# Attention stage of a three-stage kernel: each k and v load takes one head of either pair and fills one run on all 128 partitions

## The chip, the cores and the metric

The kernel runs on one core of a Trainium2 chip. The metric is the device time of one execution in microseconds (us), from the launch of the program on the core to its end, taken as the median of several executions. All arithmetic is in float32; weights and activations of the large products are split into a high and a low part, each product being three matrix products.

## The reference, cut to what matters

```python
# q, k, v: (8, 8, 576, 64)   batch, head, sequence, head dim;   phi: (8, 8, 576, 32)
a = softmax(phi, axis=2)                       # over the sequence
k_m = einsum('bhsm,bhsd->bhmd', a, k)          # 32 memory rows per head
v_m = einsum('bhsm,bhsd->bhmd', a, v)
scores = (q @ k_m.transpose(0, 1, 3, 2)) / sqrt(64)
x = softmax(scores, axis=-1) @ v_m             # attention output, then (4608, 512)
h = x @ w_in;  x = (h * sigmoid(1.702 * h)) @ w_out        # 512 -> 2048 -> 512
# then: each of 4608 tokens goes to the best of 8 experts (512 -> 1024 -> 512),
# scaled by its gate probability and by a sigmoid output gate
```

## The kernel before, in words

Three stages follow each other. Stage A is attention, stage B the 512-2048-512 layer with the routing decision, stage C the experts. The change is in stage A alone.

Stage A works on 64 heads (8 batches of 8) in `NG` = 16 groups of `HG` = 4 heads. A group needs four inputs. `ph` is phi, 128 partitions of 576 floats. `qraw` is q, 128 partitions of 1152 floats. `kvm` holds k and v: its shape is `[128, 2, 2, 576]`, and its dimensions are partition, k or v (`w`), which head of a pair (`h2`), and 9 sequence rows of 64 floats (`CA * D` = 576). Partitions 0 to 63 hold heads 0 and 1 of the group (the first pair), partitions 64 to 127 hold heads 2 and 3 (the second pair). Of a head's 576 sequence rows, partition p of its half has rows 9p to 9p + 8, which lie side by side in memory: 2304 bytes. All three tiles exist twice (`u` = 0 or 1), so that group g + 2 is loaded into the buffers of group g once that group is through with them.

The loads are issued by SyncE, in program order, on one queue. For each group, `sp_group` (L456) first calls `load_phi` for group g + 2 (L415, it waits until DVE has transposed phi of the group that had the buffer, `s_phT`), then `load_qkv` (L420). `load_qkv` waits until the sums of group g are done (`s_kv`), issues two loads of k and two of v (L426), each with 64 partitions and two runs per partition, waits for the transposes of q (`s_qtr`), and issues the load of q (L429). Four chunks of w_in (L434) are loaded between the first groups. The semaphore of a `kvm` buffer rises by 16 per load, and by 64 per group.

On TensorE, `group` (L608) does this for each group: 18 transposes of the exponentials of phi (L619), the first four transposes of q (`q_part`, L605, which waits for q's load), then the 72 small products that sum k and v over the sequence (L631, which wait for the four loads of k and v), the output products of group g - 2 (L590), five more transposes of q, a transpose of the k sums (L639), and the scores (L649). ScalarE does the exponentials and the copies out of the accumulation memory and issues the stores of the attention output to `xT_scratch` (L887, one of 589,824 bytes per group). VectorE does the transposes of phi and of the scores, maxima, sums and normalisation. The engines are ordered by semaphores alone.

After group 15, SyncE's queue loads the first tile of x (L413) and the weight chunks of stage B, and stage B begins with the first product at L672. Stage B and stage C keep their own loads and are not touched.

Of the kernel before, what the change touches and what calls it, by code (L numbers as in the profile page):

```python
# [33 lines left out]
HG = 4  # L34
NG = B * H // HG
CA = 9
PA = S // CA
# [54 lines left out]
def build(nc, q, k, v, phi, w_in, w_out, w_gate, w_ogate, w1, w2, cst, out):  # L92
# [15 lines left out]
    with ExitStack() as ctx:  # L108
# [29 lines left out]
        with ExitStack() as a:  # L138
# [5 lines left out]
            qraw, kvm, ph = [], [], []  # L144
# [84 lines left out]
        s_kvl = [sem(f"kv_loaded{u}") for u in range(2)]  # L229
# [160 lines left out]
        def wait(eng, s, value):  # L390

            if not isinstance(value, int) or value > 0:
                eng.wait_ge(s, value)
# [15 lines left out]
        def _(sp):  # L409
# [10 lines left out]
            def load_qkv(g, b, u):  # L420

                wait(sp, s_kv, g - 1)
                for w, src in enumerate((k_v, v_v)):
                    for hh in range(2):
                        heads = src[bass.ds(g * HG + 2 * hh, 2)].rearrange("h (p c) d -> p h (c d)", c=CA)
                        sp.dma_start(kvm[u][hh * PA:(hh + 1) * PA, w], heads).then_inc(s_kvl[u], 16)  # L426

                wait(sp, s_qtr, 2 * (g - 1))
                sp.dma_start(qraw[u][:], q_v[bass.ds(g * P, P), :]).then_inc(s_q[u], 16)  # L429
# [11 lines left out]
            for dst, src in ((ident, "ident"), (mask, "mask")):  # L441
                sp.dma_start(dst[:], cst[src]).then_inc(s_cst, 16)
            load_qkv(0, 0, 0)
            load_phi(1, 0, 1)
            load_qkv(1, 0, 1)
            load_w(0, w_in_part(0, 0))

# [8 lines left out]
            def sp_group(g, b, r):  # L456

                u = r % 2
                if not isinstance(g, int) or g + 2 < NG:
                    load_phi(g + 2, b + 1, u)  # L460
                    load_qkv(g + 2, b + 1, u)

                if isinstance(g, int) and g + 1 < K1:
                    load_w(g + 1, w_in_part(g + 1, 0))
# [1179 lines left out]
```

## Time and profile before

| what | value |
|---|---|
| median of 3 runs | 1402.93 us |
| lowest and highest of them | 1402.65 and 1410.83 us |
| the profiled execution, its own time | 1402.57 us |
| span of its instructions | 1400.9 us |
| mean granted TensorE clock | 0.993 |
| first product of stage B (L672) starts at | 153.13 us |

The profile is of one execution on the one core. Its time is 1.67 us longer than its span, which is what lies before the first and behind the last instruction. Times in the rows are microseconds from the start of the span, unless they are marked ns. PE is TensorE, PEld its weight load, DVE VectorE, ACT ScalarE, POOL GpSimd, SPq, ACTq and POOLq the queues that issue DMAs. The DMA share is the mean busy share of the core's 16 DMA engines, and GB/s is what they moved; the records of an engine can overlap a little, so that a share can stand at 1.0 or just above.

### The profile page before, as it was taken

What the parts mean: (1) busy time and instruction counts of PE and PEld (TensorE: products, weight loads), DVE (VectorE), ACT (ScalarE), POOL (GpSimd) and SP (SyncE); (2) the same over time, 40 slices, a digit from 0 to 9 for tenths busy, and PEclk for the clock granted to TensorE, in tenths of its full rate; (3) what the DMA queues carried; (4) which work ended last, traced back from release to release, by engine and by line L of the source; (5) the groups of instructions that cost most, each with busy time, mean ns of one, the idle gap of its engine ahead of it and who ended that gap; (6) DMA issues with size and microseconds to landing.
All of it is one profiled execution on the core that took longest, in us unless ns stands there. A gap on an engine that the chain in (4) does not pass through costs nothing.

```text
span 1400.9 us, 26210 instructions
## 1 busy us (share of the span) xinstructions
PE 1351.8 (96%) x7922; PEld 1094.9 (78%) x7923; DVE 681.5 (49%) x1400; ACT 403.2 (29%) x725; POOL 517.7 (37%) x612
## 2 busy tenths in 40 slices
PE   5888899999999999999999999999999999999997
PEld 4566688888888888888888888887788888888885
DVE  4789633344353343433534344436655555555553
ACT  2455422222232232222322223223332222223221
POOL 1100486345443343433433334331434333433331
PEclk9999999999999999999999999999999999999999
DMA  9999635656556556465465654665784688649882
GB/s 229 290 325 313 234 100 168 194 200 194 181 191 183 179 169 182 171 187 175 160 183 176 179 192 147 184 189 203 236 257 119 164 254 249 185 115 261 246 237 61
DMA packets 164843, 275.31 MB, mean 197 GB/s; under 512 B 20179, under 2 KB 57316, under 8 KB 164788
## 3 DMA queue, kind: packets, MB, share of 16 engines
q1 hardware_dynamic: 104260, 197.16, 44.7%
q10 hardware_dynamic: 47408, 45.63, 12.7%
q0 software_dynamic: 13120, 31.82, 7.3%
q8 instruction: 31, 0.51, 0.2%
q14 instruction: 24, 0.20, 0.0%
HBM read 146.03 MB, written 100.45 MB: 176 GB/s over the span
## 4 chain that ended last, share of the span: by engine, by line
PE 86%; DVE 5%; DMA 3%; issue 3%; SPq 2%; ACT 0%; ACTq 0%; POOL 0%; DVEq 0%; POOLq 0%
PE ps L672 28%; PE ps L706 28%; PE ps L776 14%; PE ps L747 14%; DMA ph<-in_phi 1%; PE ps L716 1%; DMA qraw<-in_q 1%; SPq L426 1%; SPq L454 1%; PE ps L649 1%; DVE cmeta L1123 1%; DVE phT L1101 1%; DMA cq<-ch 1%; PE ps L631 0%; DMA cmeta<-record_scratch 0%
## 5 line engine op out<-in xcount | busy, mean ns | idle before, releaser
L672 PE MATMUL ps<-xs,W 128*128 (+1 forms) x1728 | 417.6, 391 | 1.1 <-DVE xs L1162 1.1
L706 PE MATMUL ps<-W,gs 128*128 128x512 f32 x1728 | 415.3, 390 | 0.1
L672 PEld LDWEIGHTS ps<-xs,W 128*128 128x128 f32 x1728 | 323.1, 188 | 72.0 <-issue 4.1
L706 PEld LDWEIGHTS ps<-W,gs 128*128 128x128 f32 x1728 | 324.3, 188 | 68.1 <-DVE gs L1217 0.8
L1215 DVE TENSOR_TENSOR gate<-ps,gate 128x512 f32<-128x512 f32 x144 | 99.6, 691 | 364.0 <-ACT gate L932 363.7
L932 ACT ACTIVATE gate<-ps 128x512 f32<-128x512 f32 x144 | 86.2, 598 | 471.3 <-PE ps L672 470.8
L776 PE MATMUL ps<-W,chT 128*128 (+1 forms) x936 | 218.3, 390 | 1.2 <-DVE chT L1348 1.2
L747 PE MATMUL ps<-W,cx 128*128 (+1 forms) x936 | 218.5, 390 | 0.5 <-issue 0.5
L1540 POOL CAST whi<-raw 128x512 fp32r<-128x512 f32 x128 | 81.3, 635 | 337.9 <-DMA raw<-in_moe_w 337.9
L776 PEld LDWEIGHTS ps<-W,chT 128*128 128x128 f32 x936 | 175.6, 188 | 38.3 <-issue 2.0
L747 PEld LDWEIGHTS ps<-W,cx 128*128 128x128 f32 x936 | 175.6, 188 | 37.3 <-issue 1.1
L1542 POOL TENSOR_TENSOR raw<-raw,whi 128x512 f32<-128x512 f32 x128 | 172.3, 1346 | 21.5 <-POOL whi L1540 20.0
L1217 DVE TENSOR_TENSOR gs<-gate,gs 128x512 fp32r<-128x512 f32 x144 | 120.4, 836 | 99.0 <-ACT gs L936 99.0
L340 POOL DMA_DIRECT2D crec<-record_scratch x160 | 90.0, 562 | 192.1 <-DMA out<-cy,cmeta 114.6
L936 ACT CAST gs<-gate 128x512 fp32r<-128x512 f32 x144 | 89.4, 621 | 115.1 <-DVE gate L1215 113.2
L997 ACT CAST chT<-cqT 128x512 fp32r<-128x512 f32 x41 | 25.2, 620 | 201.4 <-issue 159.8
L1348 DVE TENSOR_TENSOR chT<-cqT,chT 128x512 fp32r<-128x512 f32 x78 | 53.1, 691 | 38.9 <-ACT chT L997 37.6
L1312 DVE TENSOR_TENSOR cx<-cxT,cx 128x512 fp32r<-128x512 f32 x40 | 43.7, 1092 | 57.4 <-ACT cx L965 57.4
L1548 POOL DMA_INDIRECT record_scratch<-rec,posi x36 | 36.3, 1008 | 94.1 <-DVE posi L1277 85.7
L1597 POOL DMA_INDIRECT out<-cy,cmeta x39 | 43.1, 1106 | 70.5 <-ACT cy L1005 62.8
L1326 DVE TENSOR_SCALAR ch<-ps 128x512 f32<-128x512 f32 x37 | 25.5, 691 | 66.5 <-PE ps L747 66.3
L1335 DVE STREAM_TRANSPOSE cqT<-cq 128x512 f32<-128x512 f32 x78 | 50.6, 687 | 13.2 <-DMA cq<-ch 11.4
(158 smaller groups left out, 891.1 us busy)
## 6 DMA issues: line engine op xcount, KB each, us to landing
W<-expert_scratch SPq DMA_DIRECT2D x24, 2048.0 KB, 11.7
raw<-in_moe_w SPq DMA_DIRECT2D x128, 256.0 KB, 2.8
expert_scratch<-whi SPq DMA_DIRECT2D x128, 256.0 KB, 2.6
expert_scratch<-raw SPq DMA_DIRECT2D x128, 256.0 KB, 2.9
cq<-ch ACTq DMA_DIRECT2D x156, 128.0 KB, 3.9
crec<-record_scratch POOLq DMA_DIRECT2D x160, 64.0 KB, 5.6
kvm<-in_k SPq DMA_DIRECT2D x32, 288.0 KB, 5.2
kvm<-in_v SPq DMA_DIRECT2D x32, 288.0 KB, 7.0
```

Source lines behind the costliest of these rows:

```text
L340: eng.dma_start(crec[b * M:(b + 1) * M, r % 3], rows[:, b * P:(b + 1) * P].rearrange("(h n) d -> n h d", n=M)).then_inc(loaded, 16)
L672: mm = pe.matmul(ps[:, f % 2, :], W[:, col:col + P], xs[:, bass.ds(x0 + (x_lo * K1 + c) * T, T)], start=(c == 0 and w_lo + x_lo == 0), sto ...
L706: mm = pe.matmul(ps[:, 2 + s, :], gs[:, f % 2, g_lo, s * P:(s + 1) * P], W[:, col:col + DM], start=(f == 0 and g_lo + w_lo == 0), stop=(f ...
L747: mm = pe.matmul(ps[:, 3 * u + j, :], cx[:, u, x_lo, c, :], W[:, bass.ds(col, 512)], start=(c == 0 and x_lo + w_lo == 0), stop=(c == K1 - ...
L776: mm = pe.matmul(ps[:, 5 + r % 2, :], chT[:, r % 2, h_lo, c, :], W[:, bass.ds(col, DM)], start=(c == 0 and h_lo + w_lo == 0), stop=(c == C ...
L932: act.activation(gate[:, f % 2, :], ps[:, f % 2, :], ACT.Sigmoid, scale=QTOK).then_inc(b_sig, 1)
L936: act.copy(gs[:, f % 2, 0, :], gate[:, f % 2, :]).then_inc(b_ghi, 1)
L1215: dve.tensor_tensor(gate[:, f % 2, :], ps[:, f % 2, :], gate[:, f % 2, :], ALU.mult).then_inc(b_g, 1)
L1217: dve.tensor_tensor(gs[:, f % 2, 1, :], gate[:, f % 2, :], gs[:, f % 2, 0, :].bitcast(F32), ALU.subtract).then_inc(b_glo, 1)
L1348: dve.tensor_tensor(by_h(1, j), cqT[:, j * 512:(j + 1) * 512].rearrange("p (h c n) -> p h c n", h=2, n=M), by_h(0, j).bitcast(F32), ALU.su ...
L1540: pool.tensor_copy(whi[:, u, :], raw[:, u, :]).then_inc(e_hi, 1)
L1542: pool.tensor_tensor(raw[:, u, :], raw[:, u, :], whi[:, u, :].bitcast(F32), ALU.subtract).then_inc(e_lo, 1)
```

## The change

Each of the four loads of a group still moves 128 runs of 2304 bytes, 294,912 bytes in all. Before, a load was one pair: 64 partitions, and two runs (the pair's two heads) on each. Now a load is one head of either pair: the head `h2` of the first pair goes to partitions 0 to 63, the head `h2` of the second pair to partitions 64 to 127, one run on each partition. In `heads[h2]` the source's dimensions are, from the outside in, the pair (`a`, 2 of them), the partition of the pair's half (64) and the run (576 floats). The two pairs lie 73,728 floats apart, while 64 rows of 576 floats fill only 36,864, so that the outer two dimensions can't be read as one of 128. The data, the number of loads, the semaphores and the waits are the same.

```diff
                 wait(sp, s_kv, g - 1)
                 for w, src in enumerate((k_v, v_v)):
-                    for hh in range(2):
-                        heads = src[bass.ds(g * HG + 2 * hh, 2)].rearrange("h (p c) d -> p h (c d)", c=CA)
-                        sp.dma_start(kvm[u][hh * PA:(hh + 1) * PA, w], heads).then_inc(s_kvl[u], 16)
+                    heads = src[bass.ds(g * HG, HG)].rearrange("(a h) (p c) d -> h a p (c d)", a=2, c=CA)
+                    for h2 in range(2):
+
+                        sp.dma_start(kvm[u][:, w, h2], heads[h2]).then_inc(s_kvl[u], 16)
```

SyncE's queue in stage A, in the program before, the loads of group 0 and the first of group 1 (each row names the tile written, the input read, and partitions x runs x floats of the tile; x2 is two of them in a row):

```order
L418 DMA ph<-in_phi 128x576
L442 DMA ident<-const_ident 128x128
L442 DMA mask<-const_mask 128x128
L426 DMA kvm<-in_k 64x2x576 x2
L426 DMA kvm<-in_v 64x2x576 x2
L429 DMA qraw<-in_q 128x1152
L418 DMA ph<-in_phi 128x576
```

The same place in the changed program:

```order
L418 DMA ph<-in_phi 128x576
L443 DMA ident<-const_ident 128x128
L443 DMA mask<-const_mask 128x128
L427 DMA kvm<-in_k 128x1x576 x2
L427 DMA kvm<-in_v 128x1x576 x2
L430 DMA qraw<-in_q 128x1152
L418 DMA ph<-in_phi 128x576
```

No instruction has moved, on this engine or on another; only the form of the k and v loads differs, and the lines behind them are one higher.

## Rows read from the trace of the kernel before

**Rows 1.** The page: busy time by engine, and the chain that ended last.

```profile
PE 1351.8 (96%) x7922; PEld 1094.9 (78%) x7923; DVE 681.5 (49%) x1400; ACT 403.2 (29%) x725; POOL 517.7 (37%) x612
PE 86%; DVE 5%; DMA 3%; issue 3%; SPq 2%; ACT 0%; ACTq 0%; POOL 0%; DVEq 0%; POOLq 0%
```

**Rows 2.** Busy time of each engine in the two halves of stage A.

```profile
core 0: us, PE busy (x) PEld busy (x) DVE busy (x) ACT busy (x) POOL busy (x), PEclk, DMA share, GB/s
0.00:75.00 75.00, 50.81 (x950) 37.50 (x951) 46.32 (x102) 28.12 (x49) 11.34 (x18) 0.91 0.99 262
75.00:150.00 75.00, 65.05 (x1285) 45.35 (x1286) 66.74 (x151) 42.77 (x75) 0.00 (x0) 1.00 1.01 322
```

**Rows 3.** The chain that ended last, 30 to 75 us: start, length, what.

```profile
38.55 13.92 DMA qraw<-in_q
...
60.26 13.19 DMA ph<-in_phi
```

**Rows 4.** Timeline of SyncE's queue: start, length, line, transfer, count.

```profile
2.33 1.41 SPq L426 DMA_DIRECT2D kvm<-in_k  x2
...
99.48 1.43 SPq L426 DMA_DIRECT2D kvm<-in_k  x2
101.00 1.29 SPq L426 DMA_DIRECT2D kvm<-in_v  x2
102.54 0.38 SPq L429 DMA_DIRECT2D qraw<-in_q  x1
103.13 0.33 SPq L418 DMA_DIRECT2D ph<-in_phi  x1
107.44 1.43 SPq L426 DMA_DIRECT2D kvm<-in_k  x2
```

**Rows 5.** DMA issues in 0 to 150 us: count, size of each, median from issue to landing.

```profile
kvm<-in_k SPq DMA_DIRECT2D x32, 288.0 KB, 5.2
kvm<-in_v SPq DMA_DIRECT2D x32, 288.0 KB, 7.0
qraw<-in_q SPq DMA_DIRECT2D x16, 576.0 KB, 8.6
xT_scratch<-xo ACTq DMA_DIRECT2D x13, 576.0 KB, 9.2
ph<-in_phi SPq DMA_DIRECT2D x16, 288.0 KB, 9.1
raw<-in_moe_w_in SPq DMA_DIRECT2D x5, 256.0 KB, 12.9
```

**Rows 6.** The tile kvm: its instructions (duration in ns, least/median/most), and its loads' landing.

```profile
L631 PE MATMUL ps<-kvm,am x1152: 265/269/420, 13.7 to 148.8; 64*32 64x128 f32 x192
L426 SPq DMA_DIRECT2D kvm<-in_k x32: 598/608/757, 2.3 to 132.1; - x32
...
DMA to landing us min/median/max: 4.5/6.1/12.1
```

**Rows 7.** Windows (columns as in rows 2), at the end of stage A.

```profile
140.00:145.00 5.00, 4.21 (x67) 2.66 (x66) 4.44 (x13) 2.67 (x6) 0.00 (x0) 1.00 1.02 386
...
150.00:155.00 5.00, 3.82 (x33) 2.35 (x32) 4.86 (x10) 2.69 (x5) 1.78 (x2) 1.00 0.28 111
```

**Rows 8.** TensorE's timeline around the last group (start, length).

```profile
144.25 0.66 PE L605 MATMUL ps<-ident,qraw 128*128 128x128 f32 x4
145.15 2.12 PE L631 MATMUL ps<-kvm,am 64*32 64x128 f32 x66 [0.24 <-ACT am L864]
...
153.13 1.20 PE L672 MATMUL ps<-xs,W 128*128 128x512 f32 x4 [1.08 <-DVE xs L1162]
```

## The prediction

> **What bounds the kernel now.** I first read the page's busy shares and the chain that ended last [rows 1]. TensorE is busy 96% of the span and 86% of the chain is TensorE; DMA is 3% of it. So for most of its length no transfer matters. But the change touches stage A alone, the first 150 us, and an average over three stages says nothing of it. So next come the windows of its two halves [rows 2]. There the 16 DMA engines are busy 0.99 and 1.01 of the time: stage A keeps the DMA engines full from end to end. It moves 262 GB/s in the first half and 322 in the second, while VectorE is busy 46.32 and then 66.74 of 75 us. In the first half the chain waits for transfers, 13.92 us for a q and 13.19 us for a phi [rows 3]. In the second the groups follow each other every 107.44 - 99.48 = 7.96 us [rows 4], which is both what the transfers need and near what VectorE needs. The reader should take from this that stage A has no spare transfer time to give: whatever makes its loads slower lands in the total.
>
> **What a group moves.** Four k and v loads of 294,912 bytes (the 288 KB of rows 5), q with 589,824, phi with 294,912 and the store of the output with 589,824: 2,654,208 bytes, or 165,888 for each of 16 engines if they share evenly.
>
> **The change part by part.** It removes 4 loads per group and adds 4, with as many runs (128) of the same size (2304 bytes) and the same semaphore counts. No instruction moves. The issues cost SyncE 608 ns each now [rows 6], 2.4 us of a group's 7.96; even if they cost nothing, or 0.5 us more each, that hides beside the transfers, so I take 0. TensorE reads the same tile in the same order: 0. What is left is how the 128 runs are dealt out to the 16 engines.
>
> In the kernel before, every large load is led, in source and destination, by its 128 (or 64, or 32) partitions, and with those all 16 engines are full [rows 2]. The new destination has 128 partitions, but the new source is led by the pair, a dimension of 2, with 64 rows behind it, and the two can't be merged. A transfer can be dealt out only along something that source and destination both have in front. The one cut that both allow at the outermost place is in two: pair 0 (partitions 0 to 63) and pair 1 (partitions 64 to 127). I forecast that each of these loads runs on two engines, and on the same two each time, since nothing in the transfer names others. No row shows a transfer with such a source, so this is the step that carries the forecast, and I put its chance at 0.92.
>
> The Trainium skill ("DMA: Bandwidth & Descriptors", section "Why a DMA increments its semaphore by 16 and not by 1") states it as a rule: the descriptor generator looks at the slowest dimension that isn't 1 of each access pattern and takes the largest number up to 16 that divides both, and for a queue of SyncE or ScalarE these are the lowest-numbered engines. By that rule the old form (64 and 64) gives 16 engines and the new one (2 and 128) gives 2, engines 0 and 1 each time. The trace of before agrees only in that its loads, all led by multiples of 16, fill 16 engines [rows 2].
>
> **The price of one load on two engines.** Each engine carries 147,456 bytes of each load, 589,824 bytes per group. The rate of a single engine comes from rows. At 0.28 busy the core moved 111 GB/s, so a busy engine moves 111 / (16 x 0.28) = 24.8 GB/s; at 1.02 it is 386 / (16 x 1.02) = 23.7 [rows 7]; over the second half 322 / (16 x 1.01) = 19.9, and over the first 262 / (16 x 0.99) = 16.5 [rows 2]. I take 24.8, because 14 engines will stand nearly idle, which is like the window at 0.28 and unlike the full ones; 19.9 is kept as the far end.
>
> Per group the two engines then need 589,824 / 24.8 = 23.8 us for k and v, 36,864 / 24.8 = 1.5 for their sixteenth of q, 0.7 for phi and 1.5 for the store: 27.5 us against 7.96 now. This can't hide. Two groups of buffers are loaded ahead, so while a group computes, the next one's k and v are already queued, and the two engines never run dry: stage A becomes their queue. What a group computes between its landing and the next issue (about 4 us up to the last product of L631) lies beside it.
>
> **The sum.** The first k load is issued at 2.33 us [rows 4] and I let its first bytes move 2 us later: 4.3. Sixteen groups of k, v, q and phi: 16 x 26.0 = 416.4. Thirteen stores of earlier groups come in before the last q [rows 5]: 13 x 1.5 = 19.3. Four chunks of w_in at 16,384 bytes per engine and the small constants: 3.0. Landing of the last q, 1.5. That is 444.5 us, and with the four q transposes of 0.66 us and what lies around them the last group's k and v products start at about 445.5, where they now start at 145.15 [rows 8]. The difference is 300.4. From there to the first product of stage B it is 153.13 - 145.15 = 8.0 us now; the tile of x is queued behind the last q on the same two engines (65,536 bytes, 2.6 us), so that I add 1 us. Stages B and C are as they were. 1402.57 + 300.4 + 1.0 = 1704.0 us, from the profiled execution's own time, which is 0.36 below the median of the runs; I predict 1704. TensorE's clock is granted at 0.91 in the first half of stage A [rows 2] and will be low there again while it waits; that is hidden behind the transfers, and a low start of stage B would add some us at most.
>
> **Rivals.**
> *Two engines, but at the crowded rate.* The rate of 24.8 GB/s may not be had when a single engine writes 64 partitions one after the other, or when the queue that issues stalls behind a full ring. At 19.9 GB/s a group's k, v, q and phi take 645,120 / 19.9 = 32.4 us, 16 of them 518.7, the stores 13 x 1.85 = 24.1, w_in 3.7, with 4.3, 1.5 and 1.0 around: 553.3, or 408 us more than 145.15. It gives 1402.6 + 408 + 1 = 1812. For it speaks that the engines never moved more than 19.9 for long in stage A; against it, that there all 16 were full.
>
> *All 16 engines, and better placed: faster.* If the transfer is dealt out by its 128 partitions, nothing is lost, and each engine has partitions of its own, where now two halves are written in turn. The first half's 262 x 75 = 19.65 MB at the second half's 322 GB/s would take 61.0 us, 14.0 less, and the second half can give at most 75 - 66.74 = 8.3 before VectorE is the bound. That is 22 us less: 1381. For it speaks that the first half moves less than the second at a full share of engine time; against it, that the source doesn't have 128 rows in one dimension. It decides if the cut goes by the destination alone.
>
> The Trainium skill's page "SBUF — State Buffer", section "Summary: rules for kernel authors", says that a DMA-bound transfer should use 128 partitions, and that 64 reach no more of the ports than 32. By that page alone the change would gain, and this rival is the one it argues for; that 64-partition loads moved 322 to 386 GB/s here [rows 2, 7] sets no such limit on them while other loads run beside them.
>
> *No change.* Either the loads are dealt to 16 engines and the total rate is the memory's, not the placement's (1403), or each load goes to two engines but to another pair each time. Then one lands 147,456 / 24.8 = 5.9 us and some 3 of latency after its issue, 8.9 where the median is now 6.1 [rows 6], with a group of 7.96 us loaded ahead: the first group a few us later, 1406.
>
> **How the numbers follow.** Two engines at about the clean rate: 0.80. Two engines at the crowded rate: 0.12. All 16, faster: 0.03. No change: 0.05. Slower by over 1% is the first two, 0.92; within 1%, which is about what a measurement of this kernel can tell from no change, 0.05; faster 0.03. The range goes down from 1704 by the stores and w_in, 22 us, if these fit into gaps of the two engines: 1682. Upward it takes in the crowded rate, 1812.
>
> **What would show it.** In the profile after: the median landing of a kvm load between 20 and 40 us instead of 6.1; the loads of phi issued some 27 us apart; a DMA share in stage A of about (2 x 27.5 + 14 x 3.7) / (16 x 27.5) = 0.24 with 2.65 MB / 27.5 us = 97 GB/s; the chain up to 445 us mostly DMA, and TensorE waiting for q at L606 each group; the first product of stage B at about 454 us, and from there the old distances. If kvm loads land in under 8 us and the DMA share stays near 1, the cut in two is wrong. If the share is 0.24 but the groups are 34 us apart, only the rate is.

## The result and the profile after

The changed kernel takes 1700.91 us (median of 4 runs, 1696.59 to 1703.26). The kernel before, measured in the same runs, takes 1406.88 us (4 runs, 1402.65 to 1413.60). The ratio is 1.2081, with a 95% interval of 1.2016 to 1.2146: slower by a fifth. 1704 was forecast, with a range of 1682 to 1812. The profiled execution took 1698.78 us against 1402.57. All ratios below are of fast executions; one of the ten of the kernel cut by pair (2734.01 us, at a granted clock of 1.0) was a slow one, and nothing here explains it.

TensorE's timeline says where the time went. These are the first q transposes of three groups in the middle of stage A, then those of the last group and the first products of stage B (start, length, and the idle time before with its releaser):

```profile
195.62 1.12 PE L606 MATMUL ps<-ident,qraw 128*128 128x128 f32 x4 [17.73 <-DMA qraw<-in_q]
222.19 1.11 PE L606 MATMUL ps<-ident,qraw 128*128 128x128 f32 x4 [17.02 <-DMA qraw<-in_q]
248.99 1.12 PE L606 MATMUL ps<-ident,qraw 128*128 128x128 f32 x4 [17.12 <-DMA qraw<-in_q]
...
438.00 1.11 PE L606 MATMUL ps<-ident,qraw 128*128 128x128 f32 x4 [18.16 <-DMA qraw<-in_q]
...
447.20 3.01 PE L673 MATMUL ps<-xs,W 128*128 128x512 f32 x12 [1.08 <-DVE xs L1163]
```

Here the groups are 26.6 and 26.8 us apart. From the first group's q transposes at 30.43 us to the last group's at 438.00 it is 27.2 us a group on average, and in the middle, from 168.71 to 410.36 us, 26.9 us, where it was 7.96 [rows 4]. In each of these groups TensorE waits 17 to 18 us for q. Stage B begins at 447.20 instead of 153.13 [rows 8], 294.1 us later. From there to the end of the span it is 1697.1 - 447.2 = 1249.9 us, against 1400.9 - 153.1 = 1247.8 before. The whole loss, but for 2 us, is in stage A.

What the DMA engines did in it, in windows (busy time of PE, PEld, DVE, ACT and POOL with counts, granted clock, DMA share, GB/s), answers to rows 2 and 7. The last row is a stretch in which only k and v loads were under way:

```profile
75.00:150.00 75.00, 26.41 (x416) 18.97 (x418) 20.69 (x46) 12.93 (x22) 5.64 (x6) 0.64 0.30 104
...
150.00:225.00 75.00, 21.65 (x342) 15.82 (x340) 18.64 (x38) 11.65 (x20) 0.00 (x0) 0.61 0.29 103
...
218.50:223.50 5.00, 1.31 (x12) 0.97 (x16) 0.33 (x1) 0.17 (x1) 0.00 (x0) 0.50 0.13 52
```

The share of 1.01 is now 0.29, and in the window of k and v loads alone it is 0.13: two engines of sixteen are 0.125. They move 52 GB/s, so 26 GB/s each. VectorE, busy 66.74 of 75 us before, is busy 18.64. No engine of the core is near its limit, and neither are the DMA engines on average; a mean over 16 engines hides that two of them are full. The share of 0.29 also tells what the others did: if two were busy all the time, the other 14 were busy for (0.29 x 16 - 2) / 14 = 0.19 of it, an estimate of 5.1 us a group.

Where the queue stands, by SyncE's timeline for one group (start, length, transfer), which answers to rows 4:

```profile
212.78 6.81 SPq L427 DMA_DIRECT2D kvm<-in_k  x2
219.70 11.16 SPq L427 DMA_DIRECT2D kvm<-in_v  x2
231.13 6.78 SPq L430 DMA_DIRECT2D qraw<-in_q  x1
238.59 0.33 SPq L418 DMA_DIRECT2D ph<-in_phi  x1
```

The issues of two k and two v loads, 2.7 us together before, take 18 us. An issue now lasts as long as a load takes on its two engines: the chain of work from 198 to 231 us has the pieces 5.54, 5.52 and 5.54 us, all at L427, and 147,456 bytes at 26 GB/s are 5.7. I read this as a full ring, the ring being the list of transfers that have been issued and not yet moved: a new one gets in when an old one is through. No view shows the ring itself. By the same reading the page's chain, which had 2% of SyncE's queue, now has 24%:

```profile
PE 72%; SPq 24%; DMA 1%; issue 1%; DVE 1%; ACTq 0%; ACT 0%; POOL 0%; DVEq 0%; POOLq 0%
```

The reader should see that "SPq 24%" isn't a slow SyncE. It is the waiting of loads behind loads, written down under the engine that issues them.

The tile kvm, which answers to rows 6:

```profile
L632 PE MATMUL ps<-kvm,am x1152: 269/417/419, 31.5 to 442.7; 64*32 64x128 f32 x192
L427 SPq DMA_DIRECT2D kvm<-in_v x32: 3460/5578/9253, 3.7 to 413.4; - x32
```

The median issue of a v load takes 5578 ns. The k and v products take 417 ns each instead of 269, since the granted clock of TensorE is at its lower level of 1.2 GHz (0.50 in the window above) after the 17 us without work. That costs 2 us of a group (4.07 us for the 72 products, at 223.23 us, against 2.17 before) and lies beside the transfers.

### The profile page after: what moved, and what is told of

Its sections match the earlier page's. It is cut to its first block, busy times and chain, and to the rows that moved or that the text cites. A ratio compares the mean times of both kernels' runs of the same rounds, so it can differ in the third digit from the quotient of the medians.

```text
span 1697.1 us, 26210 instructions
## 1 busy us (share of the span) xinstructions
PE 1378.2 (81%) x7922; PEld 1115.0 (66%) x7923; DVE 676.6 (40%) x1400; ACT 405.5 (24%) x725; POOL 516.6 (30%) x612
## 4 chain that ended last, share of the span: by engine, by line
PE 72%; SPq 24%; DMA 1%; issue 1%; DVE 1%; ACTq 0%; ACT 0%; POOL 0%; DVEq 0%; POOLq 0%
PE ps L673 23%; PE ps L707 23%; SPq L427 17%; PE ps L777 12%; PE ps L748 12%; SPq L430 5%; DMA qraw<-in_q 1%; SPq L418 1%; PE ps L717 1%; SPq L455 1%; ACTq L991 0%; PE ps L632 0%; DMA cq<-ch 0%; PE ps L591 0%; DVE chT L1349 0%
## 5 line engine op out<-in xcount | busy, mean ns | idle before, releaser
L606 PE MATMUL ps<-ident,qraw 128*128 128x128 f32 x144 | 30.1, 351 | 291.9 <-DMA qraw<-in_q 291.9
L606 PEld LDWEIGHTS ps<-ident,qraw 128*128 128x128 f32 x144 | 19.9, 175 | 300.1 <-DMA qraw<-in_q 238.9
L1102 DVE STREAM_TRANSPOSE phT<-ph 128x576 f32<-128x576 f32 x16 | 12.5, 778 | 274.9 <-DMA ph<-in_phi 274.9
L1516 POOL CAST W<-raw 128x512 fp32r<-128x512 f32 x16 | 10.9, 679 | 311.8 <-DVE xs L1163 303.4
L876 ACT COPY qT<-ps 128x512 f32<-128x512 f32 x16 | 9.4, 585 | 278.6 <-PE ps L606 278.6
## 6 DMA issues: line engine op xcount, KB each, us to landing
W<-expert_scratch SPq DMA_DIRECT2D x24, 2048.0 KB, 11.4
```

## The experiments

Nine runs, in the order in which they were made. In each, k and v come in four loads a group unless it is said otherwise, and the mark is the start of the first product of stage B in the one profiled execution of each kernel: 153.13 us in the kernel before, 447.20 in the changed one. The first four were executed once each, the others 6 to 12 times; the kernel before ranges from 1398.56 to 1420.06 us beside them. In the diffs a minus is a line of the changed kernel, and `...` stands for what is left out.

### Half of the loads: k in the new form, v in the old

```diff
-                for w, src in enumerate((k_v, v_v)):
-                    heads = src[bass.ds(g * HG, HG)].rearrange("(a h) (p c) d -> h a p (c d)", a=2, c=CA)
+                heads = k_v[bass.ds(g * HG, HG)].rearrange("(a h) (p c) d -> h a p (c d)", a=2, c=CA)
...
+                for hh in range(2):
+                    heads = v_v[bass.ds(g * HG + 2 * hh, 2)].rearrange("h (p c) d -> p h (c d)", c=CA)
+                    sp.dma_start(kvm[u][hh * PA:(hh + 1) * PA, 1], heads).then_inc(s_kvl[u], 16)
```

> Only k is loaded in the new form; v is loaded as before, by pair on 64 partitions. Theory 1 (a load runs on as many engines as its leading dimension allows, here the same two): per group two loads of 5.7 us instead of four on the two engines, v's sixteenth 1.4 us, and the 3.9 us of the rest: 16.8 us per group against 26.8. Stage B's first product near 287 us, total near 1541 us. Rival (any load in the new form holds up the queue of all, whatever its bytes): the pace stays near 26.8 us and the total near 1700 us.

Measured: 1567.0 us, mark at 317.20, and the groups 18.7 us apart. The loss falls with the number of loads in the new form, as theory 1 has it and the rival doesn't. But the pace is 1.9 us above what was expected. Windows of this kernel say why: a stretch with k loads alone, one in which everything else moves, and again k alone.

```profile
100.00:105.00 5.00, 3.86 (x60) 3.30 (x64) 2.19 (x3) 1.22 (x2) 1.88 (x2) 0.52 0.14 53
106.00:113.00 7.00, 3.79 (x66) 2.29 (x62) 4.50 (x9) 3.26 (x5) 0.00 (x0) 1.00 1.02 282
113.50:119.00 5.50, 0.00 (x0) 0.00 (x0) 0.00 (x0) 0.00 (x0) 0.00 (x0) 0.64 0.14 54
```

The two kinds of transfer take turns. While v, q, phi and the store move (2,064,384 bytes), all 16 engines are full, and go at 282 GB/s, not at the clean rate at which I had priced v's sixteenth: 7.3 us. With 11.4 us for the two k loads that is 18.7, the pace that was measured.

### The source led by four, and by eight

The destination, the number of loads, the runs and the bytes stay; only the number that leads the source changes.

```diff
-                    heads = src[bass.ds(g * HG, HG)].rearrange("(a h) (p c) d -> h a p (c d)", a=2, c=CA)
+                    heads = src[bass.ds(g * HG, HG)].rearrange("h (p c) d -> h p (c d)", c=CA)
                     for h2 in range(2):
-
-                        sp.dma_start(kvm[u][:, w, h2], heads[h2]).then_inc(s_kvl[u], 16)
+                        sp.dma_start(kvm[u][:, w, h2], heads[:, 32 * h2:32 * h2 + 32]).then_inc(s_kvl[u], 16)
```

> k and v loads whose source is led by the group's four heads, 32 rows of each, on the same 128 partitions, with the same number of loads, runs and bytes (the rows land on other partitions than the sums need, so k and v sums differ from the reference's). Theory 1: four engines, a load 2.9 us on each, 11.4 + 3.9 = 15.3 us per group, first product of stage B near 263 us, total near 1517 us. Rival (it is the 128-partition destination with one run each that is slow, whatever leads the source): as the changed kernel, 447 us and 1700 us.

Measured: mark at 275.04, pace 16.0 us, total 1557.27.

```diff
-                    heads = src[bass.ds(g * HG, HG)].rearrange("(a h) (p c) d -> h a p (c d)", a=2, c=CA)
+                    heads = src[bass.ds(b * H, H)].rearrange("h (p c) d -> h p (c d)", c=CA)
                     for h2 in range(2):
-
-                        sp.dma_start(kvm[u][:, w, h2], heads[h2]).then_inc(s_kvl[u], 16)
+                        at = 16 * (2 * w + h2)
+                        sp.dma_start(kvm[u][:, w, h2], heads[:, at:at + 16]).then_inc(s_kvl[u], 16)
```

> As led_by_four, but the source is led by the batch's eight heads, 16 rows of each (again other rows than the sums need; bytes, runs and loads are the same). Theory 1: eight engines, 1.4 us a load, 5.7 + 3.9 = 9.6 us per group if the engines keep their clean rate, 11 us if they are crowded; first product of stage B at 172 to 195 us, total 1426 to 1448 us. Rival (destination): 447 us and 1700 us.

Measured: mark at 191.96, pace 11.2 us, total 1427.51.

Windows from 75 to 150 us, first of the one led by four, then of the one led by eight:

```profile
75.00:150.00 75.00, 42.09 (x676) 30.02 (x666) 35.97 (x78) 23.14 (x39) 1.89 (x2) 0.73 0.52 174
```

```profile
75.00:150.00 75.00, 55.48 (x936) 38.99 (x933) 50.08 (x109) 31.64 (x54) 0.00 (x0) 0.86 0.75 247
```

With 2, 4, 8 in front of the same 128 partitions the share is 0.30, 0.52, 0.75 and the pace 26.9, 16.0, 11.2 us. Take 4 loads x 294,912 bytes at 26 GB/s per engine, 22.7, 11.3 and 5.7 us for 2, 4 and 8 engines, and the rest of a group is 4.2, 4.7 and 5.5 us: the rest grows as it gets more crowded, and theory 1 stands. (26 GB/s was measured with two engines; that four and eight keep it is taken, not shown.) This is what the rival of the 128-partition destination can't give. The mark of the first is 12 us later than expected, which is again the rest at the crowded rate; the second fell inside its span of 172 to 195 us. The totals are of no use here. The sums differ, so tokens go to other experts, and from the mark to the end of the span it is 1280.6 us in one and 1233.8 in the other, against 1247.8; I ought to have written the expectations for the mark alone.

### The same two engines, or one slow queue?

Theory 1 says that every such load goes to the same two engines. A queue that serves one such load after the other would look the same, as long as all come from SyncE. So v was issued by ScalarE, which has a queue of its own, once its copy in a group has shown that the buffer is free; SyncE's queue keeps k, as in the first experiment:

```diff
...
+            def load_v(g, u):
+
+                heads = v_v[bass.ds(g * HG, HG)].rearrange("(a h) (p c) d -> h a p (c d)", a=2, c=CA)
+                for h2 in range(2):
+                    act.dma_start(kvm[u][:, 1, h2], heads[h2]).then_inc(s_kvl[u], 16)
...
                 a_out(g)
+                if not isinstance(g, int) or 1 <= g < NG - 1:
+                    load_v(g + 1, 1 - u)
...
+            load_v(0, 0)
+            load_v(1, 1)
```

> The changed kernel, but the two v loads of a group are issued by ScalarE on its own queue. Theory 1 (the same two engines serve every such load, from whichever queue): pace 26.8 us per group, total 1700 us within 20. Rival (what is slow is SyncE's queue, which serves one such load after the other): two queues side by side, 11.4 + 3.9 = 15.3 us per group, total near 1517 us.

Measured: 1702.77 us, mark at 442.76, with TensorE's q transposes of two neighbouring groups at

```profile
250.33 1.11 PE L604 MATMUL ps<-ident,qraw 128*128 128x128 f32 x4 [18.31 <-DMA qraw<-in_q]
277.00 1.11 PE L604 MATMUL ps<-ident,qraw 128*128 128x128 f32 x4 [17.98 <-DMA qraw<-in_q]
```

26.7 us apart, as with one queue. Two queues didn't share the work. That they fill the same two engines is seen directly where loads of both queues were out at once (ScalarE issued two v loads from 259.22 to 265.67 us, SyncE two k loads from 262.07 to 275.15):

```profile
266.00:274.00 8.00, 0.00 (x0) 0.00 (x0) 0.00 (x0) 0.40 (x1) 0.00 (x0) 0.50 0.13 51
```

The share is 0.13 there and not 0.25. The profile doesn't say which two of the 16 they are.

### Each new load cut in two by pair

```diff
-                    heads = src[bass.ds(g * HG, HG)].rearrange("(a h) (p c) d -> h a p (c d)", a=2, c=CA)
-                    for h2 in range(2):
-
-                        sp.dma_start(kvm[u][:, w, h2], heads[h2]).then_inc(s_kvl[u], 16)
+                    for hh in range(2):
+                        heads = src[bass.ds(g * HG + 2 * hh, 2)].rearrange("h (p c) d -> h p (c d)", c=CA)
+                        for h2 in range(2):
+                            sp.dma_start(kvm[u][hh * PA:(hh + 1) * PA, w, h2], heads[h2]).then_inc(s_kvl[u], 16)
...
-                wait(pe, s_kvl[u], 64 * (b + 1))
+                wait(pe, s_kvl[u], 128 * (b + 1))
```

> Each load of the changed kernel is cut in two, one head on 64 partitions: eight loads per group, each source led by 64 rows, one run per partition. Theory 1: 16 engines again, and the time of the kernel before, 1403 us, up to 1412 us because SyncE issues eight loads (5 us of a group's 8). Rival (loading one head per instruction, one run on a partition, is what costs): above 1440 us.

Measured: ratio to the kernel before 1.0004 (0.9975 to 1.0034), median of its ten executions 1410.69 against 1407.66; mark at 156.09. With 64 in front of the source the loss is gone. One run per partition and one head per load cost nothing, and twice the number of issues costs 3 us at the mark and nothing that the total can tell.

### 128 partitions with a source led by 128

Two neighbouring heads are one stretch of memory, so their 128 rows are one dimension. For this, half 0 must hold heads 0 and 2 and half 1 heads 1 and 3, and the sums of head h take half h % 2 and slot h // 2. The weights that they are multiplied with come out of the transposes at L620, so these must put heads 0 and 2 on the first 64 partitions. In the first version each head is transposed by itself, 36 products of 32 rows instead of 18 of 64, and the two slots stand in two banks of the accumulation memory.

```diff
-                    heads = src[bass.ds(g * HG, HG)].rearrange("(a h) (p c) d -> h a p (c d)", a=2, c=CA)
                     for h2 in range(2):
-
-                        sp.dma_start(kvm[u][:, w, h2], heads[h2]).then_inc(s_kvl[u], 16)
+                        heads = src[bass.ds(g * HG + 2 * h2, 2)].rearrange("h (p c) d -> (h p) (c d)", c=CA)
+                        sp.dma_start(kvm[u][:, w, h2], heads).then_inc(s_kvl[u], 16)
...
-                    for hh in range(2):
-                        rows = slice(hh * PA, (hh + 1) * PA)
-                        tr = pe.matmul(ps[rows, c // 8, (c % 8) * 2 * M:(c % 8 + 1) * 2 * M], aT[rows, c * PA:(c + 1) * PA],
-                                       ident[rows, rows], start=True, stop=True, tile_position=(hh * PA, hh * PA))
+                    for h in range(HG):
+                        rows, mem = slice(h % 2 * PA, (h % 2 + 1) * PA), slice(h * M, (h + 1) * M)
+                        tr = pe.matmul(ps[rows, h // 2, c * M:(c + 1) * M], aT[mem, c * PA:(c + 1) * PA],
+                                       ident[mem, mem], start=True, stop=True, tile_position=(h * M, h % 2 * PA))
...
-                        hh, h2 = h // 2, h % 2
+                        hh, h2 = h % 2, h // 2
...
```

> Each load takes two neighbouring heads, whose 128 rows of 2304 bytes are one stretch of memory and merge into one leading dimension of 128; so the destination is 128 partitions as in the changed kernel. The transposes of the exponentials are cut by head (36 of 32 rows instead of 18 of 64) so that the sums stay as they were. Theory 1: 16 engines, stage B's first product at 131 to 153 us, total 1381 to 1403 us: the gain of up to 22 us if spreading over all partitions helps the first half of stage A. Rival (a 128-partition destination is slow by itself): 1700 us. Second rival (the transposes' extra instructions sit on the path of each group, 0.6 us each): 1403 to 1413 us.

Measured: ratio 0.9959 (0.9934 to 0.9984), median 1400.45 against 1407.66; mark at 150.93. So a 128-partition destination isn't slow. The DMA issues of this kernel in 0 to 150 us, beside those of the kernel before (which were not among the rows above):

```profile
q1 hardware_dynamic: 17856, 35.86, 73.3%
...
kvm<-in_k SPq DMA_DIRECT2D x32, 288.0 KB, 4.0
kvm<-in_v SPq DMA_DIRECT2D x32, 288.0 KB, 5.4
```

```profile
q1 hardware_dynamic: 17856, 35.86, 85.7%
```

As many packets and bytes took 73.3% of the 16 engines' time instead of 85.7, and the loads land in 4.0 and 5.4 us where it was 5.2 and 7.0 [rows 5]. 12.4% of 16 x 150 us over the 64 x 128 runs is 36 ns for each run of 2304 bytes, if all of it is put down to the k and v loads; the packets of q and phi, which gain from a less crowded queue too, are in the same row. That is the gain of the rival "all 16 engines, and better placed", which the changed kernel could not have.

To price the 36 transposes, the same loads ran with the 18 old ones, so that k and v of heads 1 and 2 change places.

> The loads of neighbours with the transposes as before, so that k and v of the group's second and third head change places (routing then differs, so the first product of stage B is the mark, not the total). It prices the extra transposes: if they cost nothing, the mark is that of neighbours within 1 us; if they sit on the path, it is up to 10 us earlier. Against the kernel before (153.1 us) it shows what 128 partitions on 16 engines give by themselves: theory 1 with the gain expects 131 to 145 us, without it 150 to 154 us.

Measured: mark at 141.70, 11.4 us before that of the kernel before, and 9.2 before that of the version with 36 transposes (the total, ratio 1.0093, has another routing in it). The windows that show what the 36 cost are below, under the last one.

### Both at once: 18 transposes that pick their heads

A transpose here is a product with the unit matrix, and its columns choose what comes out. If all 128 rows of the exponentials are read and the columns of heads 0 and 2 (or 1 and 3) are taken, 18 products give the order that is wanted. The loads, and the line `hh, h2 = h % 2, h // 2`, are those of the version before.

```diff
                     for hh in range(2):
                         rows = slice(hh * PA, (hh + 1) * PA)
-                        tr = pe.matmul(ps[rows, c // 8, (c % 8) * 2 * M:(c % 8 + 1) * 2 * M], aT[rows, c * PA:(c + 1) * PA],
-                                       ident[rows, rows], start=True, stop=True, tile_position=(hh * PA, hh * PA))
+                        pick = ident[:].rearrange("p (j k m) -> p k j m", j=2, k=2)[:, hh]
+                        tr = pe.matmul(ps[rows, c // 8, (c % 8) * 2 * M:(c % 8 + 1) * 2 * M].rearrange("p (j m) -> p j m", j=2),
+                                       aT[:, c * PA:(c + 1) * PA], pick, start=True, stop=True, tile_position=(0, hh * PA))
```

> The loads of neighbours, but the sums kept right with 18 transposes as before: each reads all 128 rows of the exponentials and picks the columns of two heads (0 and 2, or 1 and 3) out of the unit matrix. Theory (128 partitions on 16 engines gain 11 us in stage A, and the 36 transposes of neighbours cost most of it): stage B's first product near 142 us, total near 1391 us, faster than the kernel before by 0.8%. Rival (the transposes cost nothing, since they take 1.25 us per group either way, and the 9 us between neighbours and neighbours_swapped are scatter of single executions or a wait at one place): first product anywhere from 141 to 151 us, and the total as neighbours within 0.3%.

Measured: 1391.34 us against 1408.39, ratio 0.9900 (0.9871 to 0.9929); mark at 142.19. It beats both kernels, by 1.0% the one before. (The profiled execution, at 1398.68 us, was the slowest of the six; its mark is in stage A and stands.) The two halves of stage A, which answer to rows 2:

```profile
0.00:75.00 75.00, 57.15 (x1094) 41.72 (x1095) 55.87 (x124) 33.78 (x59) 11.02 (x18) 0.95 0.92 310
75.00:150.00 75.00, 65.97 (x1196) 45.87 (x1194) 66.63 (x142) 43.68 (x74) 6.73 (x8) 1.00 0.88 296
```

The first half moves 310 GB/s instead of 262, and VectorE does 55.87 us of work in it instead of 46.32. In the second half the DMA share falls from 1.01 to 0.88 and yet nothing goes faster: from 118.69 to 126.65 us two groups are 7.96 us apart, as before. So nearly the whole gain is in the first half, and in the second the transfers, though their engines were full, did not set the pace.

> neighbours once more, beside neighbours_18 on the same chip, to see whether its first product of stage B stands at 151 us in a second execution. Theory: 151 us and 1400 us. Rival (scatter): another value between 141 and 151 us.

Measured: ratio 0.9971 (0.9951 to 0.9992), median 1403.49, mark at 150.80. The mark is where it was, so the 9 us aren't scatter. One stretch holds most of them. Windows from 49 to 66 us, of the version with 36 transposes and of the one with 18:

```profile
49.00:66.00 17.00, 13.49 (x195) 9.17 (x186) 9.58 (x25) 5.45 (x10) 0.00 (x0) 0.60 0.63 231
```

```profile
49.00:66.00 17.00, 14.51 (x288) 10.08 (x287) 15.71 (x36) 9.46 (x18) 0.00 (x0) 1.00 0.98 322
```

And TensorE's timeline of the first (36 transposes):

```profile
52.82 1.33 PE L590 MATMUL ps<-pT,vbd 64*128 64x288 f32 x4 [3.51 <-issue]
```

TensorE stands 3.5 us without a releaser in the trace at 49.3 us, and then has its lower clock for a group and a half. The second execution has the same 3.49 us before the same product, at 51.0. The 36 transposes of a group take 1.25 us, as the 18 do, so it isn't their time. Why TensorE stops there is not settled: I didn't try to shift it.

## Why the prediction was right

**The cut in two.** This was the step with no row behind it, and it held: 0.13 of 16 engines in a stretch of k and v loads, the series 2, 4, 8, and 64 and 128 in front restoring the old time or better. That the two engines are the same for every load, which I took without a row, was shown by the share of 0.13 while two queues had loads out. The sentence of the Trainium skill that gave this rule ("DMA: Bandwidth & Descriptors", section "Why a DMA increments its semaphore by 16 and not by 1") agrees with each of these runs: 2, 4 and 8 are what divides both sides, and 16 where 64 or 128 leads both. That the engines are the lowest-numbered ones no run here shows.

**The rate.** The clean 24.8 GB/s per engine was taken, from a window in which the engines were mostly idle, over the 19.9 of the full ones. Measured were 26, so that a load takes 5.7 us instead of 5.95. For four loads that is 22.7 instead of 23.8 us. The rival with the crowded rate (1812) falls: two engines among idle ones don't feel the crowd.

**The rest of a group.** Its q, phi and store were priced at 3.7 us, and 26.9 - 22.7 leaves 4.2 for them. The 14 other engines, which were to be busy for 3.7 us a group, were so for about 5.1. That is why the DMA share came out at 0.29 and 0.30 and not at the 0.24 that was to be seen. In the changed kernel the error is small. In k_only, where v came on top, the same step was off by 1.9 us per group, because transfers on 16 engines come in bursts that go at the crowded rate while the two-engine loads wait.

**Nothing hides it.** 27.2 us per group on average against a forecast of 27.5, mark at 447.2 against 454.5. The queue never ran dry. In the kernel before SyncE waited 51.6 us in all for the k and v sums, and after the change it has no such row:

```profile
SPq L426 <- PE ps L631: 51.6, 12, 5.8
```

That its issues would be held for 5.5 us each I had only as a doubt in a rival; it cost nothing, as loads lay behind it all the time. It did change one sign: the chain up to 445 us was to be mostly DMA, and it is mostly SyncE's queue. TensorE's low clock lay beside the transfers as said.

**The sum.** 300.4 + 1 were forecast and 294.1 + 2.1 came, in the profiled executions. The terms err in opposite directions. Up to the last q, forecast for 444.5 us and used from 438.00, the 16 groups of k and v loads were too dear by 17.5 us (380.5 against 363.0), and all the rest too cheap by 11 (64.0 against 75.0). That these cancel in part is luck. So is some of the 3 us between 1704 and 1700.91: the kernel before was at 1406.88 in these runs, not at the 1402.57 from which the sum starts, and between the profiled executions the forecast is 5.2 us too high. (16 x 26.0 is 416.0 and not 416.4, which changes nothing.)

**What I looked for and did not find.** The landing time of a kvm load was to be 20 to 40 us. The profile gives none for them after the change, so this sign stays unseen. The landing of q, 17.4 us at the median where it was 8.6 [rows 5], has to stand for it.

**The rule about 128 partitions.** The rival that the Trainium skill's page "SBUF — State Buffer" (section "Summary: rules for kernel authors") argues for was right about the placement and wrong about this change. Where 128 partitions are reached by all 16 engines, the runs are about 36 ns shorter and stage A 11 us, half of the 22 that I had given it as the most. I had written that rows 2 and 7 set no such limit on loads of 64 partitions. They reach 322 to 386 GB/s, but the neighbours kernel moved the same bytes in less engine time, so the 64 partitions did cost something that the rate alone didn't show.

**What bounded stage A before.** I had called it bound by transfers from end to end, with 7.96 us a group in the second half as what the transfers need. The last kernel shows this for the first half alone: with cheaper transfers the second half kept its 7.96 us. The chain that ended last in the kernel before says the same: from 80 to 150 us no transfer stands in it. Of the 14.0 us that I had offered the rival in the first half, 9.3 were had by the eighth group (its q transposes start at 70.95 us in the last kernel and at 80.25 in the one before), and the 8.3 us of the second half were not to be had from loads. For this change it made no difference, since 27 us a group are far above either bound.

## What to carry to other kernels

Before a load is reshaped, look at what leads its source as well as its destination: the number of DMA engines was the largest divisor, up to 16, that both had in front, and the destination's 128 partitions didn't help when the source was led by 2. If DMA share is far below 1 and yet everything waits for transfers, compare it with 1/16, 2/16, 4/16 in a stretch where only the suspected loads move, and suspect a queue that "issues" for microseconds (here 5.5 instead of 0.6) of waiting behind its own loads. If 128 partitions are wanted from pieces that don't merge, change which pieces go together until they are one stretch, and pay for the new order where it is cheap, here in the columns of a unit matrix.

## What the runs showed of the hardware that I had not expected

An issue of a two-engine load was held for 5.5 us, the time of one load on its engines. A load of q landed 17.4 us after its issue, so that about three such loads (3 x 5.54 = 16.6 us) lay ahead of it; this is an estimate. Two DMA engines moved 26 GB/s each, and 17.6 each (282 / 16) when all 16 were full of mixed loads. A DMA share of 1.01 didn't mean that transfers set the pace: at 0.88 the groups still came every 7.96 us. And TensorE stopped for 3.5 us at the same place in two executions of the kernel with 36 transposes, in the first with a granted clock of 0.60 over 17 us, and not in the one with 18.
